# k's cast on ScalarE, routing steps spread anew, and the passage to the first expert tile reordered in an attention kernel with two expert layers

## The chip, the cores and the metric

One Trainium2 chip, one core. The metric is the device time of one execution in microseconds (us). The profile is one execution; all times of its rows count from its span's start.

## The reference

Decayed causal attention, then two layers that send each token to one of eight experts.

```python
batch, n_heads, seq, head_dim = (4, 8, 576, 64)
...
scores = scale * np.matmul(q, k.transpose(0, 1, 3, 2))
decay = cum[:, :, :, None] - cum[:, :, None, :]   # cum = cumsum(log(clip(f, 1e-4, 1)))
scores = np.where(causal, -1000000000.0, scores + decay)
attn = softmax(scores)                            # row maximum taken off, + 1e-9 in the divisor
x = (attn @ v)                                    # as 2304 tokens x 512
...
logits = (x / |x|) @ (emb / |emb|).T / tau        # layer 1; layer 2: x @ w_gate
expert_idx = argmax(logits);  gate_w = its softmax probability
out[mask] = gate_w[mask, None] * (np.maximum(x[mask] @ w1[e], 0.0) @ w2[e])
```

N = 2304 tokens, D = 512, E = 8 experts, F = 1024.

## The kernel before, in words

Five engines run lists written out by hand and meet at counting semaphores. f32 products are made from parts: each operand is split into a leading part in fp32r and the remainder, and three products are added.

**Attention.** The loop `for h in range(HEADS)` runs over 32 heads in each engine's list; b = h // 8 is the batch, hh = h % 8 the head in it. In iteration h TensorE works by key on head h (`by_key`, L408 to L416, `weighted`, L432, `back(h - 1)`, L440) and by query on head h+1 (`by_query`, L403 and L404), whose row minima VectorE takes (`mins`, L868) and TensorE lays into a row (`minima_row`, L422). ScalarE copies that row into the operand (`row_in`, L678); `by_key(h + 1, 0)` waits for it. ScalarE's list in an iteration: `keep_ot(h - 1)` (L683), `exps(h, 0)` to `exps(h, 2)` (L672), `leading_q(h + 2)` (L666), `exps(h, 3)`, `exps(h, 4)`, squares of the batch before (`g_square`, L686), the exponentials of routing (`route_exp`, L694), in odd heads from 17 on a weight chunk's cast (`split_hi`, L703), then `row_in(h + 1)`. VectorE's list: `leading_k(h + 2)` (L828, the cast of k), one step of routing for the batch before (`routing_step`), `mins(h + 1, 4)` and `mins(h + 1, 3)`, `rest_k(h + 2)` (L840), the other three `mins`, `rest_q(h + 2)` (L834), `norm(h - 1)` (L904 to L919: divisors from `back`'s product, the head's share of the logits, the head's rows of x, the sum of the logits), and in odd heads from 17 on `split_lo` (L1089). GpSimd copies the leading parts of k and q (`copy_k(h + 2)`, L1292, first in its iteration; `copy_q`, L1287), clears the diagonal blocks (`clear`, L1299) and stores table entries by indirect DMA (`scatter`, L1340).

**SyncE's queue** is the order of the loads, and the diff does not touch it. Iteration h: wait for remainders and copies of head h, load q and k of head h+2 (L292, L293, two halves each, two buffers), cumulative sums of head h+2 (L297), wait for `pv_done >= h` (the products of head h-1), load v of head h+2 (L301); for even h from 16 on one chunk of the first expert's weights (L311, L315; 512 KB); for h % 4 == 2 and h > 4 two stores of finished rows (L319, L321). So q and k of head h+3 are issued after v of head h+2 and what follows it.

**Routing** of a batch (in the iterations of the next one): largest logit and its expert (`largest_batch`, `choose_batch`, L972 to L984), ranks within the expert by a product with a triangle of ones (`g_ranks`, L462 to L467; `read_ranks`, `place_batch`), entries (`enter_batch`, L1015 to L1018), one-hot matrices of the first 256 slots (`key_batch`, `hot_batch`, L1024 and L1029), scaling by the norm (`scale_batch`, with GpSimd's root in `norms`, L1333), gates (`gate_batch`, L1077 to L1079) and their three bf16 parts (`parts_batch`, L1036 to L1040).

**The passage.** Behind the last head the last batch is routed in one go. TensorE keeps busy with `warm_up` products (L481) between its short steps, and makes the first two tiles' tokens from the one-hot matrices (`first_slots`, L474). `first_tokens(0)` gives 128 rows' numbers; GpSimd's list then has: `norms(B - 1)`, the gather of these rows (L1403), five scatters, two stores that store nothing (`store_y(0, 1)`, `store_entries(1)`), and per tile `rows_of` (the next tile's numbers, L1371, and gather, L1379; it waits for `ent_kept` and `x_turned`), `store_y` and `store_entries`. SyncE loads the second expert's weights, eight chunks, when the first gather has landed. TensorE turns the rows (`turn_rows`, L445) and ScalarE and VectorE split them (L759, L1195).

**Expert layers.** `tile_loop` runs over tiles of 128 tokens of each expert: products with w1 (L607), relu and turn, products with w2 (L636), 21 tiles in layer 1 and 22 in layer 2. The next tile's rows are turned in the middle of a tile, so TensorE waits there for their gather.

## Time and profile before

| | us |
|---|---|
| three runs | 904.73, 910.94, 911.35 (median 910.94) |
| the profiled execution | 905.14, its span 903.6 |
| TensorE busy | 862.4 (95%) |
| VectorE busy | 575.3 (64%) |
| ScalarE busy | 403.8 (45%) |
| GpSimd busy | 293.9 (33%) |
| chain that ended last | TensorE 80%, VectorE 11%, DMA 3%, issue 3% |

Stretches of the span: 0 to 29 start and head 0, 29 to 268 heads 1 to 30, 268 to 304 head 31 and the passage, 304 to 588 the first expert layer, 588 to 608 between the layers, 608 to 904 the second. A row of the timeline gives start and duration, the engine, the line, the operation, output and inputs, shapes, count, and in brackets the engine's idle time before and what ended it. Rows of stretches give, for each engine, busy time and number of instructions, then TensorE's granted clock (1.00 is full), the DMA engines' busy share and GB/s.

### The profile page before, as it was taken

What the parts mean: (1) busy time and instruction counts of PE and PEld (TensorE: products, weight loads), DVE (VectorE), ACT (ScalarE), POOL (GpSimd) and SP (SyncE); (2) the same over time, 40 slices, a digit from 0 to 9 for tenths busy, and PEclk for the clock granted to TensorE, in tenths of its full rate; (3) what the DMA queues carried; (4) which work ended last, traced back from release to release, by engine and by line L of the source; (5) the groups of instructions that cost most, each with busy time, mean ns of one, the idle gap of its engine ahead of it and who ended that gap; (6) DMA issues with size and microseconds to landing.
All of it is one profiled execution on the core that took longest, in us unless ns stands there. A gap on an engine that the chain in (4) does not pass through costs nothing.

```text
span 903.6 us, 16352 instructions
## 1 busy us (share of the span) xinstructions
PE 862.4 (95%) x5025; PEld 709.3 (79%) x5026; DVE 575.3 (64%) x1723; ACT 403.8 (45%) x708; POOL 293.9 (33%) x459
## 2 busy tenths in 40 slices
PE   6999999999997899999999999969999999999995
PEld 5788777777776788888888888858888888888884
DVE  7777888888876576757487767536652264425643
ACT  2455645646652553535265535205551254324541
POOL 7344455345435422233133222222122121122120
PEclk7999999999999999999999999989999999999998
DMA  4334444544522854334265544306652162516100
GB/s 133 95 103 128 128 123 131 152 141 126 169 63 72 296 172 170 124 129 160 98 206 172 169 156 136 113 26 227 217 187 95 35 226 69 189 41 223 46 26 23
DMA packets 59244, 119.63 MB, mean 132 GB/s; under 512 B 11934, under 2 KB 20638, under 8 KB 59204
## 3 DMA queue, kind: packets, MB, share of 16 engines
q1 hardware_dynamic: 49620, 96.93, 33.2%
q0 software_dynamic: 9440, 22.18, 7.5%
q8 instruction: 19, 0.31, 0.1%
q14 instruction: 21, 0.17, 0.1%
q10 hardware_dynamic: 144, 0.04, 0.0%
HBM read 104.13 MB, written 17.99 MB: 135 GB/s over the span
## 4 chain that ended last, share of the span: by engine, by line
PE 80%; DVE 11%; DMA 3%; issue 3%; SPq 1%; POOL 1%; ACT 0%; POOLq 0%; DVEq 0%; ACTq 0%
PE ps L636 27%; PE ps L607 26%; PE ps L445 8%; PE ps L432 5%; PE ps L440 4%; DVE ps L868 3%; PE ps L450 2%; PE ps L403 2%; PE ps L415 2%; PE ps L416 1%; PE ps L404 1%; DVE kA L840 1%; DMA k_raw<-in_k 1%; DVE kA L828 1%; DVE hot L1029 1%
## 5 line engine op out<-in xcount | busy, mean ns | idle before, releaser
L1089 DVE TENSOR_TENSOR wlo<-stage,whi 128x1024 fp32r<-128x1024 f32 x136 | 160.0, 1221 | 31.8 <-ACT whi L703 30.3
L703 ACT CAST whi<-stage 128x1024 fp32r<-128x1024 f32 x136 | 133.6, 1057 | 0.0
L768 ACT ACTIVATE h_s<-ps 128x512 f32<-128x512 f32 x44 | 26.3, 598 | 219.9 <-PE ps L607 219.9
L432 PE MATMUL ps<-probT,v_s 128*65 128x448 f32 (+4 forms) x384 | 103.3, 391 | 3.5 <-POOL probT L1299 3.4
L636 PE MATMUL ps<-whi,hT_hi 128*128 128x512 f32 x352 | 99.5, 404 | 0.0
L636 PE MATMUL ps<-whi,hT_lo 128*128 128x512 f32 x352 | 99.1, 403 | 0.0
L607 PE MATMUL ps<-whi,xT_hi 128*128 128x512 f32 x352 | 94.9, 392 | 3.0 <-DVE xT_lo L1195 3.0
L607 PE MATMUL ps<-whi,xT_lo 128*128 128x512 f32 x352 | 95.2, 392 | 0.0
L636 PE MATMUL ps<-wlo,hT_hi 128*128 128x512 f32 x352 | 95.0, 392 | 0.0
L607 PE MATMUL ps<-wlo,xT_hi 128*128 128x512 f32 x352 | 94.9, 392 | 0.0
L868 DVE CUSTOM_DVE_ANT_0 ps<-ps,maskf 128x576 f32<-128x576 f32 (+4 forms) x160 | 75.3, 510 | 20.6 <-PE ps L404 19.2
L672 ACT ACTIVATE probT<-ps 128x576 f32<-128x576 f32 (+4 forms) x160 | 66.2, 435 | 41.8 <-PE ps L416 38.1
L607 PEld LDWEIGHTS ps<-whi,xT_hi 128*128 128x128 f32 x352 | 65.7, 188 | 18.2 <-ACT xT_hi L759 3.5
L636 PEld LDWEIGHTS ps<-wlo,hT_hi 128*128 128x128 f32 x352 | 66.2, 188 | 14.7
L607 PEld LDWEIGHTS ps<-wlo,xT_hi 128*128 128x128 f32 x352 | 66.1, 188 | 14.7
L607 PEld LDWEIGHTS ps<-whi,xT_lo 128*128 128x128 f32 x352 | 66.2, 188 | 14.2
L1227 DVE TENSOR_TENSOR hT_lo<-ps,hT_hi 128x512 fp32r<-128x512 f32 x44 | 30.4, 690 | 71.4 <-ACT hT_hi L775 71.2
L636 PEld LDWEIGHTS ps<-whi,hT_lo 128*128 128x128 f32 x352 | 63.0, 189 | 11.2
L636 PEld LDWEIGHTS ps<-whi,hT_hi 128*128 128x128 f32 x352 | 62.8, 188 | 11.1
L415 PE MATMUL ps<-qB,kB 97*128 97x288 f32 (+2 forms) x192 | 69.5, 371 | 0.3 <-ACT probT L672 0.3
L1371 POOL COPY ent_next<-ent_tab 128x4 int32 (+1 forms) x45 | 8.6, 192 | 182.8 <-DVE ent_mid L1196 181.5
L1243 DVE COPY y_idx<-ent_cur 128x1 int32<-128x1 int32 x44 | 6.7, 152 | 94.2 <-PE ps L636 94.2
(223 smaller groups left out, 1626.6 us busy)
## 6 DMA issues: line engine op xcount, KB each, us to landing
stage<-in_moe_w SPq DMA_DIRECT2D x128, 512.0 KB, 4.3
q_raw<-in_q SPq DMA_DIRECT2D x64, 144.0 KB, 3.0
k_raw<-in_k SPq DMA_DIRECT2D x64, 144.0 KB, 3.1
v_s<-in_v SPq DMA_DIRECT2D x32, 162.5 KB, 2.3
x<-o_rows SPq DMA_DIRECT2D x8, 512.0 KB, 3.9
kB<-cum_hl SPq DMA_DIRECT2D x64, 2.2 KB, 1.7
table<-entry POOLq DMA_INDIRECT x44, 2.5
table<-tinit SPq DMA_DIRECT2D x2, 288.0 KB
```

The lines of the kernel that those rows point to most:

```text
L415: pe.matmul(o, kB[a][0:ROW + 1, k0:k0 + P], qB[a][0:ROW + 1, lo:hi], start=True, stop=False)
L432: mm = pe.matmul(ps[0:D + 1, OT_AT + lo:OT_AT + hi], v_s[h % 3][:, t, :], probT[:, col:col + hi - lo], start=(t == 0), stop=(t == QT - 1 o ...
L440: mm = pe.matmul(back_ps[:, t, :], o_t[:, t * P:(t + 1) * P], i_emb[:, h % H, :], start=True, stop=True)
L445: mm = pe.transpose(bank[:, c * P:(c + 1) * P], src[:, c * P:(c + 1) * P], ident[:])
L607: mm = pe.matmul(h_ps[hf], x[:, c * P:(c + 1) * P], w1_sl(w[b], c, hf * 512, 512), start=(wi == 0 and c == 0), stop=(wi == 2 and c == DC - 1))
L636: mm = pe.matmul(y_ps, h[:, kk * P:(kk + 1) * P], w2_sl(w[b], kk), start=(hf == 0 and wi == 0 and kk == 0), stop=(hf == 1 and wi == 2 and ...
L672: act.activation(probT[0:M, PT_AT[t]:PT_AT[t] + S - t * P], ps[0:M, T_AT[t]:T_AT[t] + S - t * P], ACT.Exp, scale=-1.0).then_inc(exps_done, 1)
L703: act.copy(whi[b][:, c, :], stage[:, c, :]).then_inc(w_hi[c], 1)
L768: act.activation(h_s[:, 0:512], h_ps[0], ACT.Relu).then_inc(h_relu[0], 1)
L868: dve.tensor_tensor_reduce(out=tile, in0=tile, in1=maskf[0:M, at:at + q1], scale=1.0, scalar=LARGE, op0=ALU.add, op1=ALU.min, accum_out=sm ...
L1089: dve.tensor_tensor(wlo[b][:, c, :], stage[:, c, :], whi[b][:, c, :].bitcast(F32), ALU.subtract).then_inc(w_lo[c], 1)
L1227: dve.tensor_tensor(hT_lo[:, 0:512], hT_ps[0], hT_hi[:, 0:512].bitcast(F32), ALU.subtract).then_inc(h_lo[0], 1)
```

## The change

- `leading_k` moves from VectorE's list to ScalarE's: `leading_k(2)` in head 0 behind `leading_q(2)`, `leading_k(h + 3)` behind `exps(h, 4)`; heads 0 and 1 stay with VectorE.
- Routing steps get other heads: hot matrices in hh 5, entries in hh 4, scaling in hh 6, gates and parts together in hh 7; squares and exponentials follow on ScalarE (squares 0 in hh 1, 1 and 2 in hh 2, 3 in hh 3, 4 in hh 4, exponentials in hh 6). GpSimd's first scatter of a batch is in hh 7.
- `norm` is cut into `divisors`, `head_logits`, `head_rows`, `add_logits`; for the last head the rows come behind the choice of the experts.
- Behind the last head: ScalarE keeps the last products ahead of its squares; VectorE counts the tiles and finds the first tokens before it adds the squares; ranks and first slots of the last batch have places in PSUM of their own; TensorE turns the first gathered rows when they land, after one warm-up of 56 products, and ScalarE and VectorE split them at once; the first `keep_entry` comes later; the two empty stores of GpSimd go, and all counts of `y_out` and `ent_out` with them.

```diff
-        rk_ps = ps[:, 2 * 512 + 448:2 * 512 + 448 + QT * E]
+        rk_ps = [ps[:, n * 512 + 448:n * 512 + 448 + QT * E] for n in (2, 5)]
-        first_ps = ps[:, 2 * 512 + 496:2 * 512 + 508].rearrange("p (t c) -> p t c", t=2)
+        first_ps = [ps[:, c:c + 12].rearrange("p (t c) -> p t c", t=2) for c in (2 * 512 + 496, 6 * 512)]
...
             first_slots(B - 1, range(1), 0, 3)
-            warm_up(WARM_UP // 2)
+            warm_up(WARM_UP)
+            pe.wait_ge(xg_in, 16)
+            turn_rows(xg, x_ps).then_inc(x_turned, 1)
             pe.wait_ge(vals_done, B)
             first_slots(B - 1, range(1), 3, 6)
...
                 pe.wait_ge(tiles_done, m + 1)
-                warm_up(WARM_UP * 2 if m else WARM_UP)
-
-                pe.wait_ge(xg_in, 16 if m == 0 else tile.get(16, 16))
-                turn_rows(xg, x_ps).then_inc(x_turned, 1)
+                if m == 1:
+                    warm_up(WARM_UP * 2)
+                    pe.wait_ge(xg_in, tile.get(16, 16))
+                    turn_rows(xg, x_ps).then_inc(x_turned, 1)
...
+            def leading_k(h):
+
+                act.wait_ge(k_hi, h)
+                act.wait_ge(k_in[h % 2], (h // 2 + 1) * 32)
+                act.copy(kA[h % 3][:, 0:S], k_raw[h % 2][:]).then_inc(k_hi, 1)
...
                 exps(h, 2)
                 if h + 2 < HEADS:
                     leading_q(h + 2)
+                if h == 0:
+                    leading_k(2)
                 exps(h, 3)
                 exps(h, 4)
+                if h + 3 < HEADS:
+                    leading_k(h + 3)
                 if b > 0 and hh == 1:
                     act.wait_ge(norm_done, b * H)
                     g_square(b - 1, 0)
+                if b > 0 and hh == 2:
                     g_square(b - 1, 1)
-                if b > 0 and hh == 2:
                     g_square(b - 1, 2)
+                if b > 0 and hh == 3:
                     g_square(b - 1, 3)
-                if b > 0 and hh == 3:
+                if b > 0 and hh == 4:
                     g_square(b - 1, 4)
-                if b > 0 and hh == 5:
+                if b > 0 and hh == 6:
                     route_exp(b, b - 1)
                 if h in SPLIT_AT:
                     split_hi(0, SPLIT_AT.index(h), 1)
                 if h + 1 < HEADS:
                     row_in(h + 1)
 
+            keep_ot(HEADS - 1)
             act.wait_ge(norm_done, HEADS - 1)
-            g_square(B - 1, 0, DM - D)
-            keep_ot(HEADS - 1)
-            for t in range(1, QT):
+            for t in range(QT):
                 g_square(B - 1, t, DM - D)
             act.wait_ge(norm_done, HEADS)
...
+                act.wait_ge(x_turned, 2 if m == 0 else tile.get(1, 2))
+                act.copy(xT_hi[:], x_ps).then_inc(x_hi, 1)
                 act.wait_ge(tiles_done, m + 1)
-                xv = 2 if m == 0 else tile.get(1, 2)
-                act.wait_ge(x_turned, xv)
-                act.copy(xT_hi[:], x_ps).then_inc(x_hi, 1)
...
             def leading_k(h):
 
                 dve.wait_ge(k_in[h % 2], (h // 2 + 1) * 32)
-                if h >= 3:
-                    dve.wait_ge(t_done[QT - 1], h - 2)
                 dve.tensor_copy(kA[h % 3][:, 0:S], k_raw[h % 2][:]).then_inc(k_hi, 1)
...
+            share = o_r[:, 1, :].unsqueeze(2)
+
+            def divisors(h):
+
                 dve.wait_ge(back_done, h + 1)
                 link(dve.tensor_scalar_add(o_r[:, 0, :], back_ps[:, :, D], 1e-9))
                 link(dve.reciprocal(o_r[:, 1, :], o_r[:, 0, :]))
+
+            def head_logits(h):
+
+                lo = h // H * QT
+                part = lg_raw[:, lo:lo + QT, :] if h % H == 0 else lg_part[:]
+                link(dve.tensor_tensor(part, back_ps[:, :, D + 1:BW], share.to_broadcast([P, QT, E]), ALU.mult))
+
+            def add_logits(h):
+
+                lo = h // H * QT
+                if h % H > 0:
+                    link(dve.tensor_tensor(lg_raw[:, lo:lo + QT, :], lg_raw[:, lo:lo + QT, :], lg_part[:], ALU.add))
+
+            def head_rows(h):
+
+                b, hh = h // H, h % H
                 if hh == 0 and b >= 2:
                     dve.wait_ge(x1_stored, 64 * (b - 1))
                     dve.wait_ge(ssq_done, b - 1)
-                r = o_r[:, 1, :].unsqueeze(2)
-                lo = b * QT
-                part = lg_raw[:, lo:lo + QT, :] if hh == 0 else lg_part[:]
-                link(dve.tensor_tensor(part, back_ps[:, :, D + 1:BW], r.to_broadcast([P, QT, E]), ALU.mult))
                 dve.tensor_tensor(o_rows[b % 2][:, :, hh * D:(hh + 1) * D], back_ps[:, :, 0:D],
-                                  r.to_broadcast([P, QT, D]), ALU.mult).then_inc(norm_done, 1)
-                if hh > 0:
-                    link(dve.tensor_tensor(lg_raw[:, lo:lo + QT, :], lg_raw[:, lo:lo + QT, :], lg_part[:], ALU.add))
+                                  share.to_broadcast([P, QT, D]), ALU.mult).then_inc(norm_done, 1)
 
             def wide(ap, lo, g):
...
+            def batch_regions(b):
+
+                lo = b * QT
...
             def routing_step(b, hh):
 
                 if hh == 0 and b > 1:
@@ -1109,26 +1144,25 @@
                     largest_batch(b - 1)
                 if hh == 2:
                     choose_batch(b - 1)
+                    batch_regions(b - 1)
                 if hh == 3:
                     read_ranks(b - 1)
                     place_batch(b - 1)
+                    key_batch(b - 1)
                 if hh == 4:
-                    key_batch(b - 1)
+                    enter_batch(b - 1)
+                if hh == 5:
                     hot_batch(0)
                     hot_batch(1)
-                if hh == 5:
-                    enter_batch(b - 1)
+                if hh == 6:
                     scale_batch(b - 1)
-                if hh == 6:
+                if hh == 7:
                     gate_batch(b - 1)
-                if hh == 7:
                     parts_batch(b - 1)
 
             for h in range(HEADS):
                 b, hh = h // H, h % H
                 n, m = h + 1, h + 2
-                if m < HEADS:
-                    leading_k(m)
                 if b > 0:
                     routing_step(b, hh)
                 if n < HEADS:
@@ -1146,55 +1180,57 @@
                     embedding_rows()
                     token_columns()
                 else:
-                    norm(h - 1)
-                if h in SPLIT_AT:
+                    divisors(h - 1)
+                    head_logits(h - 1)
+                    head_rows(h - 1)
+                    add_logits(h - 1)
+                if h in SPLIT_AT and h < HEADS - 1:
                     split_lo(0, SPLIT_AT.index(h), 1)
 
             add_firsts(B - 2)
...
+            split_lo(0, SPLIT_AT.index(HEADS - 1), 1)
+            divisors(HEADS - 1)
+            head_logits(HEADS - 1)
+            add_logits(HEADS - 1)
             LAST = (B - 1) * QT
             largest_batch(B - 1)
             choose_batch(B - 1)
+            head_rows(HEADS - 1)
+            batch_regions(B - 1)
+            read_ranks(B - 1)
+            place_batch(B - 1)
+            key_batch(B - 1)
+            hot_batch(0)
+            count_tiles(0)
+            dve.wait_ge(first_done, B)
+            first_tokens(0)
+            dve.sem_inc(first_rows, 1)
             dve.wait_ge(ssq_done, B)
             dve.wait_ge(sq_last, 1)
             link(dve.tensor_reduce(ssq_b[:], sq_j[:], AX.X, ALU.add))
             link(dve.tensor_tensor(ssq[:, LAST:GT], ssq[:, LAST:GT], ssq_b[:], ALU.add))
             dve.sem_inc(ssq_done, 1)
-            read_ranks(B - 1)
-            place_batch(B - 1)
-            key_batch(B - 1)
-            hot_batch(0)
             enter_batch(B - 1)
-            dve.wait_ge(first_done, B)
-            first_tokens(0)
-            dve.sem_inc(first_rows, 1)
+            hot_batch(1)
             scale_batch(B - 1)
-            hot_batch(1)
             gate_batch(B - 1)
             parts_batch(B - 1)
...
+            def row_parts():
+                dve.tensor_tensor(xT_lo[:], x_ps, xT_hi[:].bitcast(F32), ALU.subtract).then_inc(x_lo, 1)
+
+            def keep_entry():
+                dve.tensor_copy(ent_mid[:], ent_next[:]).then_inc(ent_kept, 1)
+
+            dve.wait_ge(x_hi, 1)
+            row_parts()
             dve.wait_ge(first_done, B + 2)
-            first_gates(0)
             first_tokens(1)
             first_gates(1)
+            first_gates(0)
             link(dve.tensor_copy(ent_next[:], ent_tab[0][:, 0:4]))
             dve.sem_inc(first_rows, 1)
-
-            def x_low():
-                dve.tensor_tensor(xT_lo[:], x_ps, xT_hi[:].bitcast(F32), ALU.subtract).then_inc(x_lo, 1)
-                dve.tensor_copy(ent_mid[:], ent_next[:]).then_inc(ent_kept, 1)
-
 
             dve.memset(entry1[:], OOB).then_inc(ent_done[1], 2)
...
                 dve.memset(y_idx[:], OOB).then_inc(y_ready, 2)
-                xv = 1 if m == 0 else tile.get(1, 1)
-                dve.wait_ge(x_hi, xv)
-                x_low()
+                if m == 1:
+                    dve.wait_ge(x_hi, tile.get(1, 1))
+                    row_parts()
+                keep_entry()
                 with dve.Fori(0, E // 2) as ep:
...
                     norms(b - 1)
-                if b == 1 and hh == 6:
+                if b == 1 and hh == 7:
                     pool.wait_ge(s_init, 64)
-                if b > 0 and hh >= 6:
-                    scatter(b - 1, range(hh - 6, hh - 5))
-                if b > 1 and hh < QT - 2:
-                    scatter(b - 2, range(hh + 2, hh + 3))
-            scatter(B - 2, range(2, QT))
+                if b > 0 and hh == 7:
+                    scatter(b - 1, range(1))
+                if b > 1 and hh < QT - 1:
+                    scatter(b - 2, range(hh + 1, hh + 2))
+            scatter(B - 2, range(1, QT))
...
             scatter(B - 1, range(QT))
-            store_y(0, 1)
-            store_entries(1)
             tile.add()
             for m in range(2):
                 if m == 1:
-                    pool.wait_ge(y_out, tile.get(16, 16))
-                    pool.wait_ge(ent_out, tile.get(16, 32))
+                    pool.wait_ge(y_out, tile.get(16))
+                    pool.wait_ge(ent_out, tile.get(16, 16))
                     hold(pool)
                 pool.wait_ge(tiles_done, m + 1)
                 def tile_body(j, split, m, b):
```

## Rows read from the trace of the kernel before

**Rows 1.** Busy time by stretches: one head, heads 1 to 7, 8 to 30, the passage.

```profile
52.23:59.76 7.53, 7.53 (x54) 6.11 (x53) 5.47 (x19) 3.86 (x8) 3.12 (x7) 1.00 0.36 102
29.05:82.37 53.32, 52.96 (x360) 42.75 (x359) 38.98 (x135) 27.08 (x56) 21.83 (x49) 1.00 0.40 112
82.37:268.19 185.82, 180.49 (x1214) 141.57 (x1213) 156.57 (x503) 104.64 (x223) 86.36 (x173) 1.00 0.44 130
268.19:303.96 35.77, 26.41 (x279) 22.68 (x278) 19.15 (x83) 11.77 (x26) 18.82 (x22) 0.95 0.44 151
```

**Rows 2.** ScalarE's timeline, end of head 4 (start, duration, what, idle before and its releaser).

```profile
59.01 0.63 ACT L678 CAST qB<-ps 1x576 fp32r<-1x576 f32 x1 [2.38 <-PE ps L422]
```

**Rows 3.** VectorE's timeline, head 20.

```profile
176.28 0.17 DVE L907 TENSOR_SCALAR o_r<-ps 128x5 f32<-128x5 f32 x1 [0.64 <-PE ps L440]
...
178.71 0.45 DVE L828 CAST kA<-k_raw 128x576 fp32r<-128x576 f32 x1
...
179.27 2.12 DVE L1029 TENSOR_TENSOR hot<-slots,key 128x640 bf16<-128x640 f32 x2
...
185.71 0.17 DVE L907 TENSOR_SCALAR o_r<-ps 128x5 f32<-128x5 f32 x1 [0.64 <-PE ps L440]
```

**Rows 4.** SyncE's queue (issues), heads 5, 10 and 18.

```profile
59.98 0.34 SPq L301 DMA_DIRECT2D v_s<-in_v  x1
...
62.33 0.60 SPq L293 DMA_DIRECT2D k_raw<-in_k  x1
...
101.75 0.60 SPq L293 DMA_DIRECT2D k_raw<-in_k  x1
...
160.90 0.34 SPq L301 DMA_DIRECT2D v_s<-in_v  x1
...
165.89 0.60 SPq L293 DMA_DIRECT2D k_raw<-in_k  x1
```

**Rows 5.** Issue to landing of k: 56 issues, then those at 101.75 and 165.89.

```profile
DMA to landing us min/median/max: 2.8/3.1/4.5
...
DMA to landing us min/median/max: 2.9/2.9/2.9
...
DMA to landing us min/median/max: 4.0/4.0/4.0
```

**Rows 6.** ScalarE's timeline, heads 10 and 17.

```profile
97.08 0.63 ACT L678 CAST qB<-ps 1x576 fp32r<-1x576 f32 x1 [1.52 <-PE ps L422]
...
102.13 0.62 ACT L686 ACTIVATE squares<-o_rows 128x512 f32<-128x512 f32 x1
...
104.61 0.63 ACT L678 CAST qB<-ps 1x576 fp32r<-1x576 f32 x1 [1.16 <-PE ps L422]
...
158.32 1.03 ACT L703 CAST whi<-stage 128x1024 fp32r<-128x1024 f32 x1
```

**Rows 7.** The timeline of all engines, head 0.

```profile
24.17 0.72 POOL L1299 TENSOR_SCALAR_AFFINE_SELECT probT<-probT 128x128 f32<-128x128 f32 x2 [1.25 <-ACT probT L672]
...
24.97 0.76 PE L432 MATMUL ps<-probT,v_s 128*65 128x128 f32 x3
...
25.08 0.68 ACT L666 ACTIVATE qA<-q_raw 128x576 fp32r<-128x576 f32 x1
```

**Rows 8.** GpSimd's timeline, the passage.

```profile
281.34 1.20 POOL L1333 TENSOR_TENSOR nrm<-ssq,half 128x5 f32<-128x5 f32 x1 [3.12 <-DVEq L1162]
286.00 1.59 POOL L1403 DMA_INDIRECT xg<-x,ent_tab  x1 [3.47 <-DVEq L1170]
...
296.76 0.21 POOL L1371 COPY ent_next<-ent_tab 128x4 int32 x1
```

**Rows 9.** The chain of waits, the passage (start, duration, what).

```profile
285.23 0.78 issue
...
297.90 6.02 DMA xg<-x,ent_next
```

**Rows 10.** Busy time by stretches: the warm-up ahead of the first tile.

```profile
289.00:294.00 5.00, 4.71 (x56) 4.72 (x57) 2.50 (x19) 0.00 (x0) 3.78 (x5) 0.66 0.63 184
```

54 lines of the change are left out of this document (26 added, 28 removed).

## The prediction

> **What bounds the kernel now.** I read the table by stretches first, then ScalarE's timeline, SyncE's queue and VectorE's timeline inside single heads, then the start, and last the passage to the first expert layer. The stretches are: heads 1 to 7 in 53.3 us, heads 8 to 30 in 185.8, from head 31 to the second gather's landing 35.8 [rows 1], and then two expert layers, two thirds of the span, in which the 40 slices show TensorE at nine tenths and more. The diff changes nothing of their steady state, so what can move are the first three.
>
> A head that nothing disturbs takes 7.53 us and TensorE is busy for all of it [rows 1]. Before such a head ends, ScalarE sits idle for 2.38 us and then copies the row of minima (L678, 0.63) [rows 2]. `by_key(h, 0)` started 0.12 to 0.13 us after this copy ended in nearly every head, so there is hardly any slack behind it: a late row costs the same time on TensorE. Heads 8 to 30 would take 23 x 7.53 = 173.2 us; they take 185.8. The surplus is 12.6 us, and VectorE makes most of it. In head 20 its loop, from one `o_r` to the next, is 9.43 us: 2.43 for divisors, rows and the remainder of a weight chunk (1.28 and 1.15), k's cast and the key, two hot matrices 2.12, then the minima, and TensorE waits for the last minimum [rows 3].
>
> **VectorE's relief.** k's cast costs VectorE 0.36 to 0.46 us of each loop (178.71 to 179.07) [rows 3]. In heads where VectorE ends last I charge what stands ahead of `mins(n, 4)`, plus 2.96 to 3.2 us for minima and remainder of k, plus 1.43 for `back`. The loop passes 7.53 when the first part passes 2.9 or so. The old routing steps cost, in order of hh, about 0.2, 1.3, 1.2, 1.2, 2.3, 1.6, 1.3, 1.8 us. The new spread gives 0.2, 1.3, 1.2, 1.4, 0.95, 2.1, 0.65 and 3.05. In the last 16 heads the even ones also carry the 1.15 of the remainder of a weight chunk (it is written at the end of the odd head before). So the new surpluses are: hh 5 (hot) 0.4 in each batch; hh 7 (gate and parts, 1.28 + 3.05 + 4.39 - 7.53) 1.2 in batches 1 and 2; even heads of batches 2 and 3 about 0.3 to 0.5; and what TensorE itself adds for ranks and first slots (0.35 to 0.45) stays. They add up to 7.3. **Term 1: 7.3 - 12.6 = -5.3 us.** Bounds: -12.6 (all surplus goes) and 0.
>
> **k's cast on ScalarE.** Its price there is that of the row with the same shape, 128x576 f32 to fp32r, q's 0.68 [rows 7]; issued back to back it adds 0.60 to 0.68. ScalarE has 2.38 us to spare, so the work itself is covered. What is not covered is its wait. `leading_k(h + 3)` stands behind `exps(h, 4)` and ahead of `row_in(h + 1)`, and it waits until k of head h+3 has landed. SyncE's queue is unchanged: it issues q and k of h+3 behind v of h+2, which waits for head h-1's products. So these loads start 0.22 us after head h begins, and the landing falls inside the very head in which ScalarE now wants it. Before, VectorE wanted it only at the next head's start. In head 5, v is issued at 59.98, the last half of k at 62.33; issue to landing is 2.8 us at least, 3.1 in the median, 4.5 at most [rows 4, 5]. That puts the landing 5.1 to 6.2 us behind the head's begin; add wait and cast (0.70) and row copy and its signal (0.76). The head then ends at 6.6 to 7.7 against 7.53. Plain heads just about fit.
>
> Three kinds of head don't fit. In heads 6, 10 and 14 SyncE issues two stores of rows ahead of the loads; in heads 18, 22 and 26 a weight chunk too; and heads 12, 16, 20, 24, 28 have landings of 6.6 to 7.0 (five heads, four with a chunk). In head 10 the last k is issued at 101.75 and lands 2.9 later, 104.65, where the row copy starts at 104.61 with its head begun at 97.83; two squares of 0.62 each with their reads (1.3 together) now stand behind the cast, so the head ends at 6.86 + 0.70 + 1.30 + 0.76 = 9.6: 2.0 late [rows 4 to 6]. In head 18 v goes at 160.90, then a chunk and two stores, the last k at 165.89, and it lands 4.0 later, 9.2 behind the head's begin (160.68) [rows 4, 5]. The head ends at 9.21 + 0.70 + 1.30 + 0.76 = 12.0, against 7.53 + 0.46 that VectorE would want.
>
> I did this sum for all 28 heads. Where a head's begin was late, the loads of that head were not (they hang on the products before it), so the next head gets that time back: the landing counts from when the head could have begun. Odd heads from 17 on add 1.03 for a weight cast [rows 6], hh 3 and 4 one square (0.65), hh 6 the exponentials (0.22). Lateness beyond VectorE's and TensorE's loops: heads 6, 10, 12, 14, 16: 0.8, 2.0, 1.6, 1.7, 1.0; heads 17, 18, 20, 22: 0.3, 3.7, 0.9, 2.5; heads 24, 25, 26, 28: 0.6, 0.5, 3.0, 1.1; heads 2, 5, 9 together 0.25. **Term 2: +19.8 us.** Bounds: 0 (each landing comes in time) and 19.8 plus 8 x 0.5 if the odd heads' landings are half a us later: 24.
>
> The Trainium skill (DMA: Bandwidth & Descriptors, "Rules for kernel authors") says to issue a DMA early and wait for its semaphore late. The change moves one wait forward and leaves the issue in place, so the rule speaks against it; the rows on the queue say by how much.
>
> **Heads 0 and 1.** In head 0 the cast for head 2 now stands behind `leading_q(2)`, which ends at 25.76 [rows 7], where VectorE made it at 20.3. GpSimd's list has `copy_k(2)` first, and `clear(0, 0)`, on which `weighted(0, 0)` waits, behind it. Cast until 26.4, copy 0.66, clear 0.4: `weighted(0, 0)` starts at about 27.4 instead of 24.97 to 25.1 [rows 7], +2.35. In head 1 the copy is done before, and its 0.55 over 7.53 goes. **Term 3: +1.8.** Bounds -0.5 and +2.5.
>
> **The passage.** ScalarE copies the last products ahead of the square that waited for the rows (0.8 earlier), and logits precede rows (0.4); the count, key and first slots come 1.15 earlier, at 283.95. But `norms(B - 1)` precedes the gather in GpSimd's list and waits for the sums of squares, which VectorE now makes behind `first_tokens(0)`. The root took 1.20 us at 281.34, out of the way; now it lies between 284.8 and 286.0, and the gather, with 0.8 us from its wait to its start, begins at 286.9 instead of 286.00 [rows 8, 9]. It lands at 290.7; the rows are turned at once, and TensorE can start the first tile at 292.9 instead of 296.2. That 3.3 us is given back at the second gather. It follows five scatters of 1.29 each and, in the new order, `keep_entry`, which is now behind both first tokens and gates: 296.3. GpSimd's copy at 296.76 becomes 296.4, the gather 297.5 instead of 297.90. It took 6.02 us [rows 8, 9], I take it because eight chunks of weights load beside it, and these start with the first landing, 0.85 later than before. Thus TensorE goes on at 303.5 to 304.6 where it did at 303.96, but after some 5 us of waiting instead of 1.6. After TensorE had been without work, but for ten small matmuls, from 285.9 to 289.3, its granted clock was 0.66 in the mean of 289 to 294 [rows 10], so for 3.4 us of the 5 it was at the lower of its two levels, 1.2 GHz; that again could lose 1.7 us. **Term 4: +0.8.** Bounds -3.3 (the second gather is early enough) and +3.
>
> **Sum.** -5.3 + 19.8 + 1.8 + 0.8 = +17.1 us. The profiled execution took 905.14 us (span 903.6), so it would become 922.2. The runs shown are 904.73, 910.94 and 911.35, the profiled one is 5.8 below their median. I add the sum to the middle of the two levels, 908, and say 925.
>
> **Rivals.** (a) The loads' landings don't bite, because most come before the row is due anyway. Term 2 becomes 0 to 4: the sum is -2.7 to +1.3, about 908. For it: plain heads have 0.1 to 0.9 us to spare. Against it: heads 18 and 26, where even VectorE, a us later in its list, waited for k. It decides if the last k lands within 6.0 us of the head's begin in store heads. (b) The other side, faster: VectorE's list. All 12.6 us of surplus in heads 8 to 30 go, term 2 stays below 1, and the early tile keeps its 3.3: -12.6 + 1 + 1.8 - 3.3 = -13, about 895. It decides when no head is longer than 7.6. Against it: hh 7 holds 3.05 us of routing alone. (c) Half: only the six store heads are late, and less so, by the 1.3 of the squares in 10, 18 and 26: 13.7 - 3.9 = 9.8 for term 2, the sum +7.1, about 915. For it: the landings of heads 12 to 28 without stores spread most, and may be of this execution alone. Against it: nothing in the list lets a square go ahead of the wait. (d) TensorE's clock falls in the new waits of 2 to 4 us in heads 18, 22 and 26 as it did at 290; 3.4 us at half speed each cost 1.7, twice that if it lasts twice as long: +5 to +10, about 932. The Trainium skill (TensorE: Matmul & The Clock Gate, "Loop structure matters more than you think") calls a wait for a DMA between matmuls the way to lose the clock; the passage shows it once [rows 10], the heads, where no wait before is over 2 us, not at all.
>
> **Chances.** Forecast 0.48, (a) 0.14, (b) 0.08, (c) 0.16, (d) 0.14. Within 1% is about what a measurement can tell from no change. 1% is 9 us: forecast and (d) are slower but for a few hundredths, (c) is half and half, (a) the same, (b) faster. Faster 0.08, same 0.22, slower 0.70. The range takes in all but (b) and the far end of (d): 906 to 938; the forecast's own is 918 to 932.
>
> **What would show it.** In the profile after: the row copy (ScalarE, `qB<-ps`) directly behind the k cast in heads 10, 14, 18, 22, 26, released by the k load; head 18 near 11.7 us and head 10 near 9.6; heads 13 and 21 near 7.9; hh 7 of batches 1 and 2 near 8.7; head 0 near 12; the stretch of heads 8 to 30 near 198 us. GpSimd's root right ahead of the first gather, and a wait of 4 to 5 us before the second turn of rows. The prediction is wrong if ScalarE waits for k in no head, or if heads 18, 22 and 26 stay at 8.4.

## The result, and the profile after

| | before | after |
|---|---|---|
| median of the runs | 910.15 us (4) | 923.27 us (4: 921.68 to 924.65) |
| profiled execution, its span | 905.14, 903.6 | 921.68, 920.1 |
| chain that ended last: TensorE, DMA, SyncE's queue, VectorE | 80%, 3%, 1%, 11% | 80%, 7%, 4%, 2% |

The ratio of after to before, estimated from all their runs, is 1.0158, 95% interval 1.0125 to 1.0191 (the two medians alone give 1.0144): slower, by less than 2% and clear of the noise. The forecast was 925 (906 to 938). Between the two profiled executions it said +17.1 us; the spans differ by 16.5, the medians by 13.1. The profiled execution of before lies near the low end of its runs (904.73 to 911.35), so a difference between two traces and one between medians need not be the same.

After, its waits (engine and operation, what it waited for: us in total, times, longest):

```profile
ACT kA L675 <- DMA k_raw<-in_k: 46.3, 23, 4.5
...
PE ps L415 <- ACT qB L687: 16.0, 12, 3.4
```

And its page, the share of each engine and each line in the chain that ended last:

```profile
PE 80%; DMA 7%; SPq 4%; ACT 3%; issue 3%; DVE 2%; POOL 1%; POOLq 0%; DVEq 0%; ACTq 0%
PE ps L639 27%; PE ps L610 26%; PE ps L445 8%; PE ps L432 6%; DMA k_raw<-in_k 5%; PE ps L440 2%; PE ps L415 2%; PE ps L403 2%; SPq L292 2%; PE ps L404 2%; PE ps L416 2%; PE ps L450 2%; ACT kA L675 1%; SPq L293 1%; ACT qB L687 1%
```

ScalarE waited 23 times for a load of k, 46.3 us in all. A ScalarE that waits costs nothing by itself; the second line says that it did here: TensorE waited 12 times, 16.0 us, for the row copy (`row_in`, now L687) that stands behind this wait. In the chain VectorE has fallen from 11% to 2%, while the loads of k have risen from 1% to 5% and SyncE's queue (the issues of q and k, L292 and L293, above all) from 1% to 4%. Two things can be read there: VectorE was relieved, and what ends a head last is a transfer.

By stretches (columns as in [rows 1]), the change lies where the forecast put it. The rows are head 0, heads 1 to 7, heads 8 to 30, head 31 until the second gather has landed, and then head 11 alone:

```profile
22.24:31.22 8.98, 6.67 (x44) 4.98 (x42) 4.62 (x13) 4.39 (x9) 3.70 (x8) 0.99 0.28 81
31.22:84.88 53.66, 53.05 (x360) 42.97 (x359) 35.89 (x130) 31.92 (x63) 22.23 (x49) 1.00 0.40 112
84.88:283.62 198.74, 182.97 (x1215) 146.21 (x1213) 142.57 (x478) 118.98 (x244) 88.73 (x171) 0.97 0.42 121
283.62:318.86 35.24, 25.52 (x251) 21.42 (x249) 19.62 (x86) 11.77 (x26) 17.55 (x21) 0.90 0.43 147
109.48:118.65 9.17, 9.17 (x52) 7.14 (x52) 5.57 (x16) 5.07 (x11) 2.72 (x7) 0.81 0.24 67
```

Heads 1 to 7 need 53.66 us where they needed 53.32, heads 8 to 30 198.74 where they needed 185.82 [rows 1]. Head 31 begins at 283.62, 15.4 later than before; from there to the end of the span it is 636.5 us against 635.4. VectorE has 14 us less to do in heads 8 to 30, ScalarE 14 us more, and TensorE's clock in the mean is 0.97 instead of 1.00. The last row shows why: in head 11 TensorE is busy without a gap, at a clock of 0.81.

After's head 10 on ScalarE's timeline (start, duration, operation, idle before and its releaser):

```profile
106.88 0.67 ACT L675 CAST kA<-k_raw 128x576 fp32r<-128x576 f32 x1 [2.43 <-DMA k_raw<-in_k]
107.46 0.62 ACT L695 ACTIVATE squares<-o_rows 128x512 f32<-128x512 f32 x1
...
108.80 0.63 ACT L687 CAST qB<-ps 1x576 fp32r<-1x576 f32 x1
```
SyncE's queue in head 18 of after:

```profile
169.43 0.34 SPq L301 DMA_DIRECT2D v_s<-in_v  x1
169.80 0.43 SPq L311 DMA_DIRECT2D stage<-in_moe_w  x1
...
171.74 1.38 SPq L292 DMA_DIRECT2D q_raw<-in_q  x1
...
174.44 0.60 SPq L293 DMA_DIRECT2D k_raw<-in_k  x1
```
And ScalarE in the same head:

```profile
177.81 0.67 ACT L675 CAST kA<-k_raw 128x576 fp32r<-128x576 f32 x1 [3.72 <-DMA k_raw<-in_k]
...
179.72 0.63 ACT L687 CAST qB<-ps 1x576 fp32r<-1x576 f32 x1
```

In head 10 (begun at 100.03) ScalarE is idle for 2.43 us until k of head 13 has landed, casts it, makes two squares, and copies the row at 108.80, 8.77 behind the head's begin; in [rows 6] it was 6.78. Head 18 began at 169.67. `v` goes out at 169.43, then a weight chunk and two stores, and the last half of k at 174.44, 5.01 us behind `v`. ScalarE's cast, which waited for it, starts at 177.81; the row copy starts at 179.72 and the next head at 180.40. TensorE had nothing to do from 177.72 to 180.40.

The passage of after on GpSimd's timeline, beside [rows 8]:

```profile
300.49 1.23 POOL L1371 TENSOR_TENSOR nrm<-ssq,half 128x5 f32<-128x5 f32 x1 [6.10 <-DVEq L1212]
301.92 1.10 POOL L1441 DMA_INDIRECT xg<-x,ent_tab  x1 [0.20 <-issue]
...
311.24 0.19 POOL L1409 COPY ent_next<-ent_tab 128x4 int32 x1 [0.83 <-DVE ent_mid L1224]
```
The second gather in its chain of waits, beside [rows 9]:

```profile
312.36 6.49 DMA xg<-x,ent_next
```
And TensorE when the first and the second gather's rows have come:

```profile
305.50 0.97 PE L445 MATMUL ps<-ident,xg 128*128 128x128 f32 x4 [3.69 <-DMA xg<-x,ent_tab]
...
318.90 0.73 PE L445 MATMUL ps<-ident,xg 128*128 128x128 f32 x4 [2.63 <-DMA xg<-x,ent_next]
```

The root (L1371) lies directly ahead of the first gather, as forecast, but the gather begins 0.20 us behind it. The rows are turned as they land, at 305.50, 21.88 behind the begin of head 31 (before 25.86), and the tile's first product with weights begins 3.7 earlier than before. The second gather takes 6.49 us (before 6.02) and lands 35.24 behind that begin (before 35.72).

### The profile page after: what moved, and what is told of

It is laid out like the page before. It is cut to its first block, busy times and chain, and to the rows that moved or that the text cites. A ratio compares the mean times of both kernels' runs of the same rounds, so it can differ in the third digit from the quotient of the medians.

```text
span 920.1 us, 16309 instructions
## 1 busy us (share of the span) xinstructions
PE 865.0 (94%) x4997; PEld 713.1 (77%) x4998; DVE 559.1 (61%) x1693; ACT 424.5 (46%) x738; POOL 291.3 (32%) x457
## 4 chain that ended last, share of the span: by engine, by line
PE 80%; DMA 7%; SPq 4%; ACT 3%; issue 3%; DVE 2%; POOL 1%; POOLq 0%; DVEq 0%; ACTq 0%
PE ps L639 27%; PE ps L610 26%; PE ps L445 8%; PE ps L432 6%; DMA k_raw<-in_k 5%; PE ps L440 2%; PE ps L415 2%; PE ps L403 2%; SPq L292 2%; PE ps L404 2%; PE ps L416 2%; PE ps L450 2%; ACT kA L675 1%; SPq L293 1%; ACT qB L687 1%
## 5 line engine op out<-in xcount | busy, mean ns | idle before, releaser
L415 PE MATMUL ps<-qB,kB 97*128 97x288 f32 (+2 forms) x192 | 70.3, 375 | 16.4 <-ACT qB L687 16.0
L1337 POOL TENSOR_SCALAR_AFFINE_SELECT probT<-probT 128x128 f32<-128x128 f32 (+1 forms) x160 | 44.5, 286 | 87.1 <-ACT probT L681 82.5
```

Source lines behind the costliest of these rows:

```text
L415: pe.matmul(o, kB[a][0:ROW + 1, k0:k0 + P], qB[a][0:ROW + 1, lo:hi], start=True, stop=False)
L1337: pool.affine_select(out=block, in_=block, compare_op=ALU.is_ge, fill=0.0, base=0, pattern=[[1, M]], channel_multiplier=-1).then_inc(clear ...
```

## The experiments

All were run with the kernel before beside them. The jobs ran on different chips, on which the kernel before took 907.52 (e1 to e4), 912.51 (e5 to e8) and 909.16 (e9 to e11), so kernels are compared through the ratio to before, which is estimated from all runs and can differ from the quotient of the two medians by up to 0.2%. "Heads" is the begin of head 31 in the profiled execution, "rest" what follows to the end of the span. In them the kernel before has 268.19 and 635.4, after 283.62 and 636.5. Differences of a few us in "rest" say little: e9 and e10 run the same code behind head 31 as before does, and it took 639.9 and 638.9 us there, not 635.4.

| run | median | ratio to before [95%] | heads | rest |
|---|---|---|---|---|
| e1 k back on VectorE | 905.43 | 0.9991 [0.9972, 1.0009] | 268.09 | 634.4 |
| e2 cast behind squares | 915.49 | 1.0084 [1.0051, 1.0116] | 279.06 | 636.6 |
| e3 loads first | 907.00 | 0.9995 [0.9978, 1.0013] | 269.50 | 636.7 |
| e4 head 0 on VectorE | 918.89 | 1.0147 [1.0114, 1.0180] | 279.43 | 636.3 |
| e5 the three together | 901.79 | 0.9879 [0.9855, 0.9903] | 261.00 | 639.7 |
| e6 longer warm-up | 906.74 | 0.9934 [0.9913, 0.9955] | 261.87 | 643.4 |
| e7 passage's order | 905.16 | 0.9918 [0.9894, 0.9941] | 261.59 | 641.5 |
| e8 second gather earlier | 901.81 | 0.9890 [0.9868, 0.9913] | 259.45 | 638.9 |
| e9 wait alone | 914.80 | 1.0070 [1.0041, 1.0099] | 276.00 | 639.9 |
| e10 cast alone | 908.20 | 0.9994 [0.9975, 1.0014] | 267.79 | 638.9 |
| e11 attention alone | 903.91 | 0.9935 [0.9912, 0.9958] | 261.98 | 640.2 |

**e1: k's cast back on VectorE.** Everything else of the change stays.

```diff
--- after
+++ e1 (ScalarE's calls of leading_k taken out; in VectorE's list:)
+                if m < HEADS:
+                    leading_k(m)
                 if b > 0:
                     routing_step(b, hh)
...                 (and in leading_k the wait for t_done, as before)
```

> The changed kernel with k's cast for all heads back at the head of VectorE's list; everything else stays changed. Theory (ScalarE's wait for k makes the loss, the new spread of routing gains a little): heads 1 to 30 lose the lateness of 19.8 us and the 2.1 of head 0, and pay the cast on VectorE where it ends last, surplus 10.4 us instead of 7.3 and 12.6 before. That is some 17 us less than the changed kernel and 0 to 3 less than before: 905 to 910. Rival (the new spread of routing, or the passage, is what costs): 915 or more.

The time is that of before. So the whole loss comes with the place of k's cast, and none from the new spread of the routing steps or the passage, where the rest is 0.9 us shorter than before. A finer expectation missed: heads 8 to 30 take 186.1 us, so on a VectorE that still casts k the new spread is worth nothing. The sum of the surpluses is unmoved; heads 15, 19 and 23 take 9.01, 8.77 and 9.42 us (before 8.34, 7.88, 8.35), heads 12, 20 and 28 less.

**e9 and e10: the wait alone and the work alone.** Both are the kernel before with one thing added to ScalarE's list, between `exps(h, 4)` and the squares.

```diff
--- before
+++ e9
                 exps(h, 4)
+                if h + 3 < HEADS:
+                    act.wait_ge(k_in[(h + 3) % 2], ((h + 3) // 2 + 1) * 32)
--- before
+++ e10 (a copy of 128x576 that nothing reads, no wait)
                 exps(h, 4)
+                if h + 3 < HEADS:
+                    act.copy(<free part of squares>, maskf[:])
```

> The kernel before with nothing but ScalarE's wait for k of head h + 3 behind exps(h, 4); the cast stays with VectorE and no instruction is added to an engine. Theory (the wait is the cost, in heads whose loads land late): heads 6, 10, 14, 16, 17, 18, 22, 25 and 26 get longer, by 0.2, 1.4, 0.8, 0.3, 0.6, 2.3, 1.0, 0.8 and 1.6 us, 9 in all: 1% over before, ratio 1.010. Rival (ScalarE's work is the cost): ratio 1.000.

> The kernel before with a copy of 128x576 more on ScalarE behind exps(h, 4) in the same 29 heads, from a tile that is there from the start into a scratch place, without a wait; it computes nothing that is used. Theory: ScalarE has 0.57 us and more to spare ahead of each row copy, so the ratio is 1.000, 1.001 at most. Rival (the work is the cost): up to 29 x 0.66 = 19 us, ratio up to 1.02.

ScalarE late in head 18 of e9:

```profile
170.91 0.63 ACT L686 ACTIVATE squares<-o_rows 128x512 f32<-128x512 f32 x1 [3.81 <-DMA k_raw<-in_k]
...
172.25 0.63 ACT L678 CAST qB<-ps 1x576 fp32r<-1x576 f32 x1
```
And in head 18 of e10:

```profile
164.77 0.66 ACT L724 COPY squares<-maskf 128x576 f32<-128x576 f32 x1
...
167.69 0.63 ACT L678 CAST qB<-ps 1x576 fp32r<-1x576 f32 x1 [1.03 <-PE ps L422]
```

With the wait ScalarE stands still for 3.81 us and the row copy follows the squares at once. With the work it still has 1.03 us to spare ahead of the row copy. The work, 0.66 us in each of 29 heads, costs nothing (head 31 begins at 267.79); the wait costs 7.8 us in the trace (1.6 of it in head 27, at a low clock) and 0.7% by the ratio. On top of the old list it is less than on the new one. One reason is that VectorE was late in the same heads (head 18 took 8.74 us before and takes 10.26 in e9). The other is that in after the cast, too, stands behind the wait: in head 18 the row copy starts 1.91 us behind the end of the wait in after (177.81 to 179.72) and 1.34 in e9 (170.91 to 172.25). So the cast is free where ScalarE has time to spare (e10), and not in a head whose load lands late.

**e2: the same wait, but behind the squares and exponentials.**

```diff
--- after
+++ e2
                 exps(h, 4)
-                if h + 3 < HEADS:
-                    leading_k(h + 3)
                 ...
                 if h in SPLIT_AT:
                     split_hi(0, SPLIT_AT.index(h), 1)
+                if h + 3 < HEADS:
+                    leading_k(h + 3)
                 if h + 1 < HEADS:
                     row_in(h + 1)
```

> The changed kernel with leading_k(h + 3) behind the squares, the exponentials and the weight cast in ScalarE's list, directly ahead of row_in(h + 1). Theory (the landing sets the time, and what stands behind the wait adds to it): squares and weight casts hide in the wait, 6 us less, 917. Rival (ScalarE's work, not the landing, is what is late): no change within 2 us, since the work is the same. Rival that all of the lateness is the squares: 12 us less.

It gives 0.7% of the 1.6% back. Head 10 falls from 9.45 to 8.46 us and heads 11 and 12 from 9.17 and 8.35 to 7.56 and 7.53. Head 18 keeps its wait (11.03), and behind it head 19 takes 9.03 with the clock low for 3.4 us (7.54 in after); head 27 takes 10.56, low for 6.8 us. The squares queued behind the wait were part of its price, the landing itself the larger one.

**e3: the wait stays, the loads go earlier.** SyncE issues the weight chunk and the two stores of a head behind the next head's loads of q and k.

```diff
--- after
+++ e3
                     load_qk(h + 2)
+                if h > 0:
+                    weights_and_stores(h - 1)
                 if h + 2 < HEADS:
                     if h > 0:
                         sp.wait_ge(t_done[QT - 1], h)
                 ...
-                (the weight chunk and store_rows of this head)
```

> The changed kernel with SyncE's queue altered: the weight chunk and the two stores of rows of iteration h are issued behind the loads of q and k of iteration h + 1 instead of ahead of them. ScalarE's list stays. Theory (in heads 6, 10, 14, 18, 22, 26 and the even heads from 16 on k lands late because of what is queued ahead of it): landings come at 5.5 to 6.2 us of the head, heads 18, 22 and 26 fall from 10.2 to 11.5 to 8 to 9, in all about 12 us less, 911. Rival (the DMA engines are the limit, not the queue's order): the loads land as late as before, and the time stays within 3 us.

This is the run that settles it. SyncE's queue in head 18 of e3:

```profile
164.39 0.34 SPq L301 DMA_DIRECT2D v_s<-in_v  x1
...
167.06 0.60 SPq L293 DMA_DIRECT2D k_raw<-in_k  x1
167.70 0.58 SPq L311 DMA_DIRECT2D stage<-in_moe_w  x1
```

And its ScalarE:

```profile
170.06 0.67 ACT L680 CAST kA<-k_raw 128x576 fp32r<-128x576 f32 x1 [0.89 <-DMA k_raw<-in_k]
...
171.98 0.63 ACT L692 CAST qB<-ps 1x576 fp32r<-1x576 f32 x1
```

The last half of k is now issued 2.67 us behind `v`, where it was 5.01, and the chunk follows it. ScalarE waits 0.89 us instead of 3.72. Heads 10, 18, 22 and 26 take 7.89, 7.90, 7.57 and 7.89 us, and head 31 begins at 269.50, 14.1 earlier than in after. That is more than I expected: heads 11, 15 and 27 take 7.52, 8.36 and 8.15 where after has 9.17, 9.52 and 9.04, since without the long waits the clock never fell in e3's heads, 3.7 us. Part of what is left of the wait sits in a single head: in head 9 a load took 4.8 us from issue to landing and the head 9.37. Another part sits in heads 19, 21, 23 and 25, which take 8.96, 8.63, 8.57 and 8.75 (after 7.54, 7.55, 7.99, 7.82): k's cast starts 5.8 to 6.3 us behind their begin, and the weight cast of 1.03 still stands behind it. In e5, where k's cast is last in the list, they take 7.54, 7.77, 8.34 and 7.53.

**e4: head 0's cast back on VectorE.**

```diff
--- after
+++ e4 (ScalarE's leading_k(2) taken out; ahead of VectorE's list of a head:)
+                if h == 0:
+                    leading_k(2)
```

> The changed kernel with k's cast for head 2 alone back on VectorE; heads 3 and later stay on ScalarE. Theory: GpSimd's first copy no longer waits behind ScalarE's exponentials and q, head 0 falls from 8.99 to about 6.9 us, the total by 2.1: 921. Rival: head 0 waits for its loads or for TensorE's clock, no change.

Head 0 falls from 8.99 to 6.43 us. The ratio follows by little (1.0158 to 1.0147, well inside the intervals), though the trace has head 31 begin 4.2 earlier: 2.6 of it in head 0; heads 11 and 15, where the clock did not fall this time, give 3.1 (7.55 and 8.00), and head 19, where it did, takes 1.5 back (9.02).

**e5: e2, e3 and e4 together.**

```diff
--- after
+++ e5
     ScalarE:  ... exps(h, 4), squares, route_exp, split_hi,
+              leading_k(h + 3),
               row_in(h + 1)
     VectorE: +leading_k(2) ahead of head 0
     SyncE:    load_qk(h + 2), +weights_and_stores(h - 1), v
```

> The changed kernel with all three cures at once: loads of q and k ahead of the weight chunk and the stores in SyncE's queue, k's cast of head h + 3 directly ahead of row_in(h + 1) in ScalarE's list, k's cast of head 2 on VectorE. Theory (lateness was the landing of k plus what stood behind the wait, and head 0): of the surplus over 7.53 us per head only VectorE's 7.3 us and some 2 us of late landings are left, head 31 begins near 264 us where it did at 268.2 before: 901 us, 0.7% less than before. Rival (the landings of the plain heads, at 6 us and more, go on to cost in most heads): no better than the run with the loads first alone, 907.

It beats both kernels: 1.2% faster than before. Head 18 of e5, SyncE's queue:

```profile
159.41 0.34 SPq L301 DMA_DIRECT2D v_s<-in_v  x1
...
162.08 0.60 SPq L293 DMA_DIRECT2D k_raw<-in_k  x1
162.72 0.58 SPq L311 DMA_DIRECT2D stage<-in_moe_w  x1
```
And its ScalarE:

```profile
165.07 0.67 ACT L680 CAST kA<-k_raw 128x576 fp32r<-128x576 f32 x1 [0.25 <-DMA k_raw<-in_k]
166.33 0.63 ACT L692 CAST qB<-ps 1x576 fp32r<-1x576 f32 x1 [0.59 <-PE ps L427]
```

The chunk and the stores follow the loads, ScalarE waits for k for 0.25 us, and then 0.59 us for TensorE: the wait no longer decides. Heads 8 to 30 take 178.9 us, a surplus of 5.7 over 23 x 7.53 where before had 12.6. That is VectorE's relief, with what late landings still cost in it. In the traces head 31 begins 7.2 us earlier than before and the rest takes 4.3 longer, 2.9 less in all, where the medians differ by 10.7 (912.51 and 901.79); before was not traced on this chip.

**e6, e7, e8: the passage, on top of e5.** e6 doubles the warm-up ahead of the first turn. e7 puts the reduction of the squares ahead of `first_tokens(0)`, ten small matmuls inside the warm-up (which grows from 56 to 92 products), and `keep_entry` ahead of `row_parts`. e8 adds to e7 that the second gather stands behind two scatters instead of five.

```diff
--- e5
+++ e6
-            warm_up(WARM_UP)
+            warm_up(WARM_UP * 2)
--- e5
+++ e7 (VectorE)
             count_tiles(0)
+            (reduction of the squares, from behind first_tokens(0))
             first_tokens(0)
...
-                row_parts()
                 keep_entry()
+                row_parts()
--- e5
+++ e7 (TensorE)
-            warm_up(WARM_UP)
+            warm_up(78)
+            first_slots(B - 1, ...)
+            warm_up(14)
             turn_rows(xg, x_ps).then_inc(x_turned, 1)
-            first_slots(B - 1, ...)
--- e7
+++ e8 (GpSimd)
-            scatter(B - 1, range(QT))
+            scatter(B - 1, range(2))
+            pool.wait_ge(tiles_done, 1)
+            rows_of(0, 0, 1, 2)
+            scatter(B - 1, range(2, QT))
...                 (stores and counts of the first tile follow; its loop starts one tile later)
```

> The run e5_three_edits with the warm-up between first_slots(0) and the turn of the first rows doubled, to 112 products, so that TensorE has work until the first gather lands. Theory (the clock that falls in that wait of 3.7 us makes the first tile slow, but the second gather hides it, and only the fall behind the second wait costs): 1 to 2 us less than e5_three_edits. Rival (all of it is hidden behind the second gather): no change within 0.5 us in the trace from head 31 on.

> The run e5_three_edits with the squares' sum of the last batch ahead of first_tokens(0) in VectorE's list, and first_slots, tokens and gates of the first two tiles ahead of the turn of the first rows (warm-up of 78 and 14 products around them). Theory: the root on GpSimd no longer stands between the first tokens and the first gather, which starts 1.2 us earlier, and keep_entry comes before the rows; the second gather still follows five scatters, so it gains the same 1.2 us: 1 to 2 us less than e5_three_edits. Rival (the second gather's landing is set by the weights' transfers, not by its issue): no change.

> The run e7_passage_order with the second gather issued after two of the five scatters of the last batch instead of after all. Theory: the gather is issued 3 to 4 us earlier and TensorE's wait of 2.6 us ahead of the second turn of rows goes: 2 to 3 us less than e7_passage_order, near 897. Rival (weights' transfers set the landing): 0 to 1 us.

e6 missed: its interval lies above e5's, the second gather begins 33.16 behind head 31's begin instead of 30.82, and between the layers the clock was low for 10.2 us and again for 6.8 (e5 once, 6.8). In the passage itself, where the products were added, it was low for less time: 10.2 us in all from head 31's begin to tile 1 where e5 has 17.1 (a granted clock of 0.89 in the mean against 0.82), and tile 1's first product came at 47.07 (47.71). The time was lost between the layers, where the code is that of e5: the last tile of the first layer with the work between the layers, and the tile after it, took 35.2 and 15.3 us (e5 33.7 and 12.5). In e7 the first gather begins 18.35 behind head 31's begin (e5 20.34) and tile 1's first product 45.84 (47.71), but the two stretches between the layers took 35.6 and 14.3 us. Whether the new order gained the 1.9 is not shown: in e5 the clock was low from 269.7 for 3.4 us, inside head 31, in e7 it was not, and after has e5's order with its first gather at 18.30. In e8 the second gather begins 26.52 behind head 31's begin (e7 29.38) and tile 1's first product 42.28 (45.84); tile 1 then takes 1.5 longer. 3.4 us remain against e7 in the median, and it ends level with e5.

**e11: e5's edits to heads, the old passage.** Before with k's cast on ScalarE in e5's place, the new spread, e3's queue order and head 0 as in e4.

```diff
--- before
+++ e11
     VectorE:  routing_step as in after, leading_k only ahead of head 0
     ScalarE: +leading_k(h + 3) ahead of row_in(h + 1)
     SyncE:    load_qk(h + 2), +weights_and_stores(h - 1), v
```

> The kernel before with the attention part of the run e5_three_edits alone: k's cast on ScalarE directly ahead of row_in, loads first in SyncE's queue, routing spread anew; the passage behind the last head is the old one. Theory: head 31 begins at 261 as in that run, and from there it takes the 635.4 us of before: span 896.5, ratio 0.992. Rival (the new passage gives something): slower than e5_three_edits. If the new passage with its cold waits costs, it is 2 to 4 us faster in the trace than e5_three_edits.

The heads give what they gave in e5 (head 31 at 261.98). The expected ratio, 0.992, lies inside the interval, but the trace does not follow the sum behind it: the span is 902.1 instead of 896.5, nearly all of the difference in the rest, 640.2 instead of 635.4. From head 31 on the clock was at its lower level for 28.4 us in e11 and 32.6 in e5, where before had 18.9. What the new passage gains or loses stays open. By the traces the rest is the same with the old passage (640.2) and the new one (639.7). By the ratios e11 is slower than e5 (0.9935 and 0.9879, and the intervals do not meet), as the rival had it, but the two ran on different chips and not side by side. What sets off the falls of the clock there was not found out.

## Why the prediction was right, by its own steps

**What bounds the kernel.** Held: in the traces all of the difference but 1.1 us arose before head 31, and there in VectorE's and ScalarE's lists. The list of heads that would be late was right, and most of their sizes:

| head | 6 | 10 | 12 | 14 | 16 | 18 | 20 | 22 | 24 | 26 | 28 |
|---|---|---|---|---|---|---|---|---|---|---|---|
| forecast | 8.3 | 9.6 | 9.1 | 9.2 | 8.9 | 11.7 | 8.8 | 10.4 | 8.5 | 10.9 | 9.0 |
| after | 8.36 | 9.45 | 8.35 | 9.55 | 8.03 | 10.73 | 8.86 | 10.24 | 8.41 | 11.47 | 9.20 |

(Heads 10 and 18 as the prediction names them. The others are 7.53 plus the lateness that it gives, and from head 16 on plus 0.4, the middle of its 0.3 to 0.5 for VectorE's loop.)

**Term 1 (VectorE's relief), -5.3.** Somewhat small: e5 has a surplus of 5.7 us against 12.6, so -6.9, where the forecast had 7.3 against 12.6. And the reason it gave was half wrong. It counted new surpluses for the new spread. Heads 13, 21 and 29 were given 7.9 us and took 7.55, 7.55 and 7.56; heads 15 and 23 were given 8.7 and took 9.52 (8.36 in e3, where the clock did not fall) and 7.99. That is 2.2 us too much. e1 shows that the spread alone gives nothing (186.1 us for heads 8 to 30, 185.8 before), so it is the 0.46 us of the cast that matters. Whether the cast's move would give as much with the old spread was not run.

**Term 2 (the wait for k), +19.8.** The mechanism is shown: the wait alone costs 7.8 us on the old list (e9), the work alone nothing (e10), and earlier loads take 14.1 of the 15.4 us away with the wait still in place (e3). The size was too large. Heads 2 to 30 grew by 13.8 us (from 37.13 to 268.19 before, from 38.76 to 283.62 after) where terms 1 and 2 gave 14.5, but heads 11, 15 and 27 contain some 1.6, 1.2 and 1.5 us that are not lateness of a load: they took 9.17, 9.52 and 9.04 at a low clock. Without these 4.3 the two terms gave 9.5, five us less than forecast. With -6.9 for term 1 that leaves 16.4 for term 2, 3.4 less than its 19.8. Mis-sized were heads 12, 16 and 18, 2.6 us together, for which it took over landings of the execution before (7.04 us behind the head's begin in 12 and 16, 9.21 in 18); after had its casts start at 6.35, 6.66 and 8.14. So rival (c), which gave such landings to this one execution, was right on head 16 and by half on head 12, and wrong on 20, 24 and 28, which came about as late as forecast.

The rule of the Trainium skill (DMA: Bandwidth & Descriptors, "Rules for kernel authors"), to issue early and wait late, is what e2 and e3 did. Waiting later gave 4.6 us in the trace, issuing earlier 14.1.

**Term 3 (heads 0 and 1), +1.8.** Measured 2.13 - 0.54 = +1.6. The sign "head 0 near 12" does not follow from this term, which makes it 6.86 + 2.35 = 9.2; it took 8.99.

**Term 4 (the passage), +0.8.** Measured +1.1. That is within what the rest differs by anyway, 635.4, 639.9 and 638.9 us for the old passage in before, e9 and e10, and 634.4 to 636.7 for the new one in after and e1 to e4, so the size proves nothing. The trace shows the mechanism named: the early first tile is given back at the second gather. One step missed its size: it gave the gather 0.8 us behind the root as in [rows 9]; it needed 0.20, and began 0.49 later than before instead of 0.9. TensorE's wait for the second rows was 2.63 us instead of 5, because tile 0 ran at a low clock for 6.8 us from 305.7 and used up the other half. Behind the wait the clock was low again, for 3.4 us from 319.36, as the term allowed for. The turn 3.98 us earlier thus became a tile 1 that begins 1.1 later (44.86 against 43.72 behind head 31's begin).

**Rival (d), the clock.** It happened, in three heads (11, 15 and 27), and the sum did not have it. It had named the waits of heads 18, 22 and 26; of these only the last was followed by a fall, and two falls came behind shorter waits, in heads 10 and 14. That the forecast and the result agree to 2 us is in part luck, two errors that cancel: five us too much in terms 1 and 2, and four us of clock left out. A reader should trust the mechanism and its order of size, not that agreement. The prediction said that no wait in the heads before was over 2 us and no clock fell; after had both, but not always together, as the last section shows.

**Rivals (a) and (b).** (a) fell with the first row of the waits. (b), the faster kernel, is not this change but three edits away: e5 reaches 0.988, where (b) said 895 of 908, 0.986.

## What to carry to other kernels

A cheap operation that waits for a load, put into an in-order list ahead of what the critical engine needs, costs nothing while the load comes in time (e10: 0.66 us of work, no loss), and else the lateness of the landing, with its own duration and all that is queued behind the wait on top: read issue and landing of that load against its new place, head by head, and count what is queued ahead of it. When it doesn't fit, move small loads ahead of bulk stores in the queue and put the wait last in the list, and the same move of work turned here from a loss of 1.6% into a gain of 1.2% (with the first head's cast left where it was). Two runs, one with the wait alone (e9) and one with the work alone (e10), are the shortest way to see which half costs.

## What the runs showed of the hardware that I had not expected

The length of a wait does not say whether TensorE's clock falls behind it. TensorE's first product behind the wait of head 10 in after (idle before in brackets):

```profile
109.48 0.40 PE L415 MATMUL ps<-qB,kB 97*128 97x288 f32 x1 [1.39 <-ACT qB L687]
```
Behind the wait of head 18:

```profile
180.40 0.40 PE L415 MATMUL ps<-qB,kB 97*128 97x288 f32 x1 [2.68 <-ACT qB L687]
```

And the granted clock of the two stretches around them, third column from the end:

```profile
109.00:114.40 5.40, 4.92 (x19) 3.75 (x20) 2.73 (x8) 3.16 (x6) 1.54 (x4) 0.70 0.46 135
180.00:186.00 6.00, 5.60 (x34) 4.49 (x35) 3.53 (x12) 4.82 (x12) 2.91 (x7) 1.00 0.28 80
```

After 1.39 us without work the clock was 0.70 in the mean of 109.0 to 114.4; after 2.68 us it stayed at 1.00. At 144.10, after 1.84 us, and at 250.30, after 3.41, it fell; at 214.60, after 2.17, it did not. Nor does the same place in the program decide: ahead of head 19 TensorE waited 2.64 us in e2 and 3.12 in e4, and there the clock fell. The low stretches are at 1.2 GHz, the lower of its two levels (a granted clock of 1.00 is 2.4). The Trainium skill (TensorE: Matmul & The Clock Gate, "Loop structure matters more than you think") says that a long wait for a DMA between matmuls makes TensorE go cold; the three falls in after's heads agree in that each came behind a wait, and the rows show that a fall can follow 1.39 us and that 2.68 may pass.

The same code between the two layers took 33.4 + 12.5 us in before and after (the last tile of the first layer with the work between the layers, and the tile after it), 35.6 + 14.3 in e7, 35.3 + 14.1 in e8 and 35.2 + 15.3 in e6; in e7 the clock was low twice there, from 589.2 and from 602.9, in before once. That is up to 4.6 us between kernels that don't differ there, and 6.6 us lie between the runs of before. More work for TensorE in the passage (e6) kept the clock up there for longer, 10.2 us low instead of 17.1 in e5, and yet the low stretches between the layers, where nothing was changed, grew from 6.8 to 17.1 us in all. What decides stays open.
